# Down-projection of the MLP in three fp32r products with its split weights read back from DRAM, and nine MLP groups of two pieces

## What is computed

```python
scores = q @ k.T / sqrt(64)                      # 4 batches, 8 heads, 576 tokens, head size 64
kth = 32nd largest score of each row
scores = where(scores >= kth, scores, -1e9)
x = softmax(scores) @ v                          # laid out as 2304 tokens x 512
h = x @ w_in                                     # 512 -> 2048
g = max(h, 0) + log1p(exp(-abs(h)))              # softplus
x2 = g @ w_out                                   # 2048 -> 512
e = argmax(x2 @ w_gate); gate = softmax weight of e      # 8 experts
out = gate * (max(x2 @ w1[e], 0) @ w2[e])        # 512 -> 1024 -> 512
```

## Time and profile before

| | |
|---|---|
| Median of 3 runs | 1120.13 us (1118.76 to 1122.27) |
| Profiled execution, its own time / its span | 1119.99 us / 1118.3 us |
| Busy: PE, PEld (weight load), DVE, ACT, POOL | 1042.2, 761.5, 838.0, 658.8, 685.6 us |
| Mean granted clock of TensorE | 0.983 |
| HBM read / written | 40.12 MB / 9.70 MB |
| Mean of one: L737, L748, L754, L761 on ACT | 0.64, 0.78, 0.77, 0.69 us |
| Mean of one: L1308, L1312, L1320 (128x512) on POOL | 2.21, 1.42, 1.30 us |

### The profile page before, as it was taken

How to read it: one execution, slowest core, us unless ns; L and a number is a source line. 1 busy time by engine, 2 the same in 40 slices (tenths; PEclk the granted TensorE clock), 3 DMA queues, 4 the chain that set the end, 5 groups by cost and what they waited for, 6 DMA issues and landing times.

```text
span 1118.3 us, 20580 instructions
## 1 busy us (share of the span) xinstructions
PE 1042.2 (93%) x6728; PEld 761.5 (68%) x6729; DVE 838.0 (75%) x1838; ACT 658.8 (59%) x1313; POOL 685.6 (61%) x487
## 2 busy tenths in 40 slices
PE   3677679999999999999999999999999999999976
PEld 1455456777767767767767677677676788888864
DVE  7999998999999999999998999994036622222241
ACT  2677777777787787787777787786345111111130
POOL 4789997887887887887877788786121211112101
PEclk9879999999999999999999999999999999999989
DMA  9200011100011110000101000000314331111100
GB/s 336 92 1 1 1 52 44 43 21 1 1 29 56 43 42 1 1 20 1 58 29 62 2 1 20 1 1 20 151 40 158 127 120 48 38 38 47 38 9 19
DMA packets 26873, 50.71 MB, mean 45 GB/s; under 512 B 2656, under 2 KB 11872, under 8 KB 25760
## 3 DMA queue, kind: packets, MB, share of 16 engines
q1 hardware_dynamic: 23744, 39.87, 10.3%
q0 software_dynamic: 3040, 9.70, 2.4%
HBM read 40.12 MB, written 9.70 MB: 45 GB/s over the span
## 4 chain that ended last, share of the span: by engine, by line
PE 82%; DVE 11%; POOL 2%; ACT 2%; issue 1%; DMA 1%; DVEq 0%; POOLq 0%; SPq 0%; ACTq 0%
PE psum L531 20%; PE psum L478 8%; PE psum L443 7%; PE psum L603 7%; PE psum L513 6%; PE psum L604 6%; PE psum L605 6%; PE psum L460 6%; PE psum L515 5%; PE psum L517 5%; DVE top L976 5%; DVE work L982 4%; PE psum L552 2%; PE psum L632 1%; POOL pr L1308 1%
## 5 line engine op out<-in xcount | busy, mean ns | idle before, releaser
L1308 POOL TENSOR_SCALAR pr<-sc,top 128x576 f32<-128x576 f32 x144 | 318.7, 2213 | 38.3 <-DVE top L976 25.4
L976 DVE MAX8 top<-work 128x8 f32<-128x576 f32 x432 | 305.9, 752 | 0.0
L531 PE MATMUL psum<-wo,hT 128*128 128x512 f32 x576 | 272.3, 595 | 0.0
L982 DVE MATCH_REPLACE8 work<-top,work 128x576 f32<-128x576 f32 x288 | 212.5, 749 | 0.0
L1312 POOL TENSOR_TENSOR pr<-pr,sc 128x576 f32<-128x576 f32 x144 | 204.4, 1420 | 12.0
L1320 POOL TENSOR_TENSOR hT<-hs,ab 128x512 f32<-128x512 f32 (+1 forms) x80 | 95.0, 1187 | 151.4 <-ACT ab L807 151.3
L513 PE MATMUL psum<-x_hi,wi_hi 128*128 128x256 f32 x512 | 152.1, 297 | 0.8 <-ACT lg L833 0.7
L531 PEld LDWEIGHTS psum<-wo,hT 128*128 128x128 f32 x576 | 98.5, 191 | 68.4 <-issue 68.4
L515 PE MATMUL psum<-x_lo,wi_hi 128*128 128x256 f32 x512 | 144.6, 282 | 0.0
L517 PE MATMUL psum<-x_hi,wi_lo 128*128 128x256 f32 x512 | 144.5, 282 | 0.0
L460 PE MATMUL psum<-ident,pr 128*128 128x128 f32 (+1 forms) x720 | 105.4, 278 | 36.9 <-ACT prT L761 19.0
(11 more groups left out here) (184 smaller groups left out, 1659.7 us busy)
## 6 DMA issues: line engine op xcount, KB each, us to landing
wbuf<-in_moe_w SPq DMA_DIRECT2D x4, 2048.0 KB, 14.6
kT<-in_k SPq DMA_DIRECT2D x16, 288.0 KB, 3.0
qT<-in_q SPq DMA_DIRECT2D x16, 288.0 KB, 3.8
vtok<-in_v SPq DMA_DIRECT2D x16, 256.0 KB, 3.0
wi_raw<-in_moe_w_in SPq DMA_DIRECT2D x1, 4096.0 KB, 14.1
wo<-in_moe_w_out SPq DMA_DIRECT2D x1, 4096.0 KB, 24.6
x_rows<-x2tok SPq DMA_DIRECT2D x16, 256.0 KB, 2.2
wi_again<-in_moe_w_in SPq DMA_DIRECT2D x1, 4096.0 KB, 13.7
```

The costliest lines, as they stand in the source:

```text
L531: mm = nc.tensor.matmul(psum[:, 6 + a, :], hT[:, n % 4, part, a * P:(a + 1) * P], wo[:, f, :], start=(f == 0), stop=(f == KF - 1))
L976: nc.vector.max(top[:, at, 8 * r:8 * r + 8], sc[:, at, :] if r == 0 else work[:, t, :]).then_inc(topk_step, 1)
L982: nc.vector.match_replace(work[:, t, :], top[:, at, 8 * r - 8:8 * r], sc[:, at, :] if r == 1 else work[:, t, :], TAKEN).then_inc(topk_step, 1)
L1308: nc.gpsimd.tensor_scalar(pr[:, n % 2 * 2 + t, :], sc[:, at, :], top[:, at, TOPK - 1:TOPK], OUT, ALU.is_lt, ALU.mult).then_inc(mask_step, 1)
```

## The change

The down-projection becomes three fp32r products: the sum h is split into a high part (`h_high` on ScalarE) and a low rest (`h_low` on GpSimd), both in the step after, and w_out likewise. w_out is split in steps 1 to 4 (`split_wo`, `low_wo`), w_in now in steps 5 to 8, two units a step each. The split w_out goes to DRAM (`wo_parts`, 1 MB a unit) and comes back unit by unit into a ring of two (`load_wo`). The MLP has nine groups of two pieces, from step 10 on; eight of them run between the blocks, the ninth after them, and the steps end at 73 instead of 77. Of the masks, one tile of each even block, and both of the first eight blocks, get their comparison from a Relu on ScalarE (`cut_off`), and GpSimd only subtracts; the biases of the exponentials move from ScalarE to GpSimd. `reciprocals` come a block later on VectorE, behind the first maxima. In the last group the order of units, router and loads is new; the first expert's w1 and w2 go, in quarters, to where attention's buffers were, between the ring loads. Buffers move in SBUF, `up` uses one bank in the last group too, and the load `wi_again` falls away.

```diff
-    NA = NT - 1
+    NA = NT - 2
...
-    GROUPS = [[0]] + [[2 * g - 1, 2 * g] for g in range(1, NT // 2)] + [[NT - 1]]
+    GROUPS = [[2 * g, 2 * g + 1] for g in range(NT // 2)]
     LASTG = len(GROUPS) - 1
-    MLP_AT = 6
...
+    MLP_AT = 2 * PAIRS + 2
+    WIDE = 2 * P
...
+    FREE = MLP_AT - 2
+
+    def cuts(n):
+        return (0, 1) if n < FREE else ((0,) if n % 2 == 0 else ())
+
+    def tiles_of(n):
+        return (0, 1) if len(cuts(n)) != 1 else (1, 0)
+
+
+
+    def wo_units(i):
+        return range(2 * (i - 1), 2 * i) if 1 <= i <= UNITS // 2 else ()
+
+    def wi_units(i):
+        return wo_units(i - UNITS // 2)
...
+    wo_parts = nc.dram_tensor("wo_parts", (UNITS, P, 2, 2, DM), F32, kind="Internal").ap()
...
+            sp.dma_start(wo_raw[:], w_out.rearrange("(k p) n -> p k n", p=P)).then_inc(wo_loaded, 16)
             sp.dma_start(wi_raw[:], w_in.rearrange("(k p) f -> p k f", p=P)).then_inc(wi_loaded, 16)
-            sp.dma_start(wo[:], w_out.rearrange("(k p) n -> p k n", p=P)).then_inc(wo_loaded, 16)
             sp.dma_start(wg[:], w_gate.rearrange("(k p) e -> p k e", p=P)).then_inc(wg_loaded, 16)
 
+            def store_wo(u):
+                sp.wait_ge(wo_split, u + 1)
+                sp.dma_start(wo_parts[u], wo_ring[:, u % 2]).then_inc(wo_stored[u % 2], 16)
+
+            def load_wo(n):
+                if n < 2:
+                    for slot in range(2):
+                        sp.wait_ge(wo_stored[slot], 16 * UNITS // 2)
+                else:
+                    sp.wait_ge(h_used, n - 1)
+                sp.dma_start(wo_ring[:, n % 2], wo_parts[n % UNITS]).then_inc(wo_ready[n % 2], 16)
+
             for i in range(TAIL):
+                if up_at(i):
+                    load_wo(UNITS * up_at(i)[0] + up_at(i)[1])
...
+                for u in wo_units(i):
+                    store_wo(u)
...
+            first = UNITS * LASTG
+            for u in range(2):
+                load_wo(first + u)
...
+            for u in range(4, 8):
+                for n in ((0, 1) if u < 6 else ()):
+                    at = slice((u - 4) * 512, (u - 3) * 512)
+                    half = slice(n * KD // 2, (n + 1) * KD // 2)
+                    sp.dma_start(w1_to[:, half, at], w1_from[:, half, at]
+                                 ).then_inc(w1_first if u == 4 else w1_loaded[0], 16)
+                for n in ((0, 1) if u >= 6 else ()):
+                    at = slice((2 * (u - 6) + n) * KE // 4, (2 * (u - 6) + n + 1) * KE // 4)
+                    sp.dma_start(w2_to[:, at, :], w2_from[:, at, :]
+                                 ).then_inc(w2_first if u == 6 else w2_loaded[0], 16)
+                load_wo(first + u)
+            for a in range(2):
+                store_piece(2 * LASTG + a)
...
             def down(g, u, part):
                 n = UNITS * g + u
                 if part == 0:
                     pe.wait_ge(h_ready, n + 1)
-                    if n == 0:
-                        pe.wait_ge(wo_loaded, 16)
+                    pe.wait_ge(wo_ready[n % 2], 16 * (n // 2 + 1))
                     if u == 0 and g:
-                        pe.wait_ge(y_copied, turns_before(g))
+                        pe.wait_ge(y_copied, 2 * g)
                 f = 2 * u + part
-                for a in range(len(GROUPS[g])):
-                    mm = nc.tensor.matmul(psum[:, 6 + a, :], hT[:, n % 4, part, a * P:(a + 1) * P],
-                                          wo[:, f, :], start=(f == 0), stop=(f == KF - 1))
+                here = wo_ring[:, bass.ds(slots[n % 2], 1)].bitcast(F32R)
+                hi, lo = here[:, 0, 0, part, :], here[:, 0, 1, part, :]
+                for a in range(2):
+                    h_at = (n % 2, part, slice(a * P, (a + 1) * P))
+                    high, low = h_hi[:, h_at[0], h_at[1], h_at[2]], h_lo[:, h_at[0], h_at[1], h_at[2]]
+                    nc.tensor.matmul(psum[:, 6 + a, :], high, hi, start=(f == 0), stop=False)
+                    nc.tensor.matmul(psum[:, 6 + a, :], high, lo, start=False, stop=False)
+                    mm = nc.tensor.matmul(psum[:, 6 + a, :], low, hi, start=False, stop=(f == KF - 1))
                 if part == 1:
...
             up(LASTG, 1)
...
+            turn_tokens(LASTG - 1, NT - 4, 0)
+            turn_tokens(LASTG - 1, NT - 3, 1)
+            last_down(0)
+            logits(NT - 4, 2)
+            logits(NT - 3, 3)
             up(LASTG, 2)
+            last_down(1)
+            count_early()
             up(LASTG, 3)
-            count_early()
-            last_down(1)
...
+            last_down(2)
+            up(LASTG, 4)
+            last_down(3)
+            up(LASTG, 5)
             slots_early()
+            last_down(4)
+            up(LASTG, 6)
+            last_down(5)
             up(LASTG, 7)
-            last_down(5)
             last_down(6)
             pe.wait_ge(tables_ready, 1)
             rank_first = rank_at(0)
             turn_xs(0, 0)
             last_down(7)
...
+            e_up(0, rank_first, {(0, 2): lambda: turn_tokens(LASTG, NT - 2, 5),
+                                 (0, 3): lambda: turn_tokens(LASTG, NT - 1, 4),
+                                 (1, 1): lambda: logits(NT - 2, 3),
+                                 (1, 2): lambda: logits(NT - 1, 7)}, halves=True)
...
+            def cut_off(n, t):
+                act.wait_ge(limit_ready, sum(1 for x in range(n + 1) if cuts(x)))
+                if n >= 2:
+                    act.wait_ge(transit_full, 2 * (n - 2) + t + 1)
+                nc.scalar.activation(pr[:, n % 2 * 2 + t, :], sc[:, n % 3 * 2 + t, :], ACT.Relu,
+                                     bias=bias[:, n % 2, 1, t:t + 1], scale=-FAR).then_inc(cut, 1)
+
+            def exponentials(n, x):
+                t = tiles_of(n)[x]
                 act.wait_ge(bias_ready, n + 1)
-
...
-            def exponentials(n, t):
-                act.wait_ge(masked, 2 * n + t + 1)
+                act.wait_ge(masked, 2 * n + x + 1)
...
+            def h_high(g, u):
+                n = UNITS * g + u
+                act.wait_ge(h_summed, n + 1)
+                if n >= 2:
+                    act.wait_ge(h_used, n - 1)
+                nc.scalar.copy(h_hi[:, n % 2], hs[:, n % 2]).then_inc(h_high_ready, 1)
+
+            def split_wo(u):
+                act.wait_ge(wo_loaded, 16)
+                if u >= 2:
+                    act.wait_ge(wo_stored[u % 2], 16 * (u // 2))
+                nc.scalar.copy(wo_ring[:, u % 2, 0].bitcast(F32R), wo_raw[:, 2 * u:2 * u + 2, :]
+                               ).then_inc(wo_hi_ready, 1)
...
-                if late:
-                    normalise(i - 2, 0)
-                    normalise(i - 2, 1)
+                if up_at(i - 1):
+                    h_high(*up_at(i - 1))
                 if is_block(i + AHEAD):
                     scores_out(i + AHEAD, 0)
                     scores_out(i + AHEAD, 1)
                 if now:
-                    biases(i - 1)
-                    exponentials(i - 1, 0)
+                    for t in cuts(i - 1):
+                        cut_off(i - 1, t)
+                if late:
+                    normalise(i - 2, 0)
+                    normalise(i - 2, 1)
                 if up_at(i):
                     rectify(*up_at(i))
                 if late:
                     probs_out(i - 2, 0)
-                if up_at(i):
-                    logarithm(*up_at(i))
-                if up_at(i - 1) and up_at(i - 1)[0] == 0:
-                    split_wi(up_at(i - 1)[1])
+                if now:
+                    exponentials(i - 1, 0)
                 if late:
                     probs_out(i - 2, 1)
                 if i in TURNS:
                     turn_out(TURNS[i][1], 5)
+                if up_at(i):
+                    logarithm(*up_at(i))
                 if now:
                     exponentials(i - 1, 1)
+                for u in wo_units(i):
+                    split_wo(u)
+                for u in wi_units(i):
+                    split_wi(u)
                 if down_at(i) and down_at(i)[1] == UNITS - 1:
...
-                if is_block(n - 1):
-                    reciprocals(n - 1)
+                    if r == 0 and is_block(n - 2):
+                        reciprocals(n - 2)
...
+            def biases(n):
+                at = slice(n % 3 * 2, n % 3 * 2 + 2)
+                pool.wait_ge(topk_step, STEPS * (n + 1))
+                if n >= 2:
+                    pool.wait_ge(exp_ready, 2 * (n - 1))
+                if cuts(n):
+                    nc.gpsimd.tensor_scalar(bias[:, n % 2, 1, :], top[:, at, TOPK - 1], FAR, None,
+                                            ALU.mult).then_inc(limit_ready, 1)
+                nc.gpsimd.tensor_scalar(bias[:, n % 2, 0, :], top[:, at, 0], -1.0, None,
+                                        ALU.mult).then_inc(bias_ready, 1)
+
             def mask(n, t):
                 at = n % 3 * 2 + t
-                pool.wait_ge(topk_step, STEPS * n + STEPS - 2 + t + 1)
```

(49 more changed lines are left out.)

326 lines of the change are left out of this document (149 added, 177 removed).

## The result

The changed kernel takes 1138.0 us, median of 4 runs (1137.7 to 1139.4), against 1121.0 for the kernel before on the same chip (4 runs, 1118.8 to 1122.3): a ratio of 1.0157, interval 1.0137 to 1.0176. It is slower, as forecast (1137). The profiled execution took 1137.8 us with a span of 1136.0, where before the span was 1118.3.

What follows compares the result with a forecast made beforehand. TensorE bounds (82% of the last path), VectorE and GpSimd within 1.1 us. 1120.0 + (810.9 - 813.1) + (58.5 - 40.5) + 1.3 = 1137.1 us, forecast 1137; own range 1120 to 1150, overall 1098 to 1150.

Steps and rivals of the forecast that it cites:

- Part 1: Down-projection in fp32r on TensorE: 2.80 us a unit for 3.53, 0.73 less per step; steps 11 to 73 626 us.
- part 2: Main phase: new chain between ScalarE and GpSimd makes a pair of steps 21.1 us, steps 11 to 73 665 us.
- rival A: Main phase: VectorE sets the pace, steps 11 to 73 take 626 us, end at 1098; chance 0.21.
- Part 3: Start: weight splits lengthen the first steps, 12.9 us each for six; step 11 comes at 138, 20.6 us later.
- The sentence on the clock's worth: Start: with TensorE at 2.4 GHz throughout, it would be 2.7 us shorter and the end 1134.
- Rival B: Start also keeps VectorE's pace: 20 us less again, end at 1078; chance 0.04.
- Part 4: Ring loads of split weights: 5 us each, covered by more than 10 us, so they cost nothing.
- Rival C: Ring loads or stores come late, or the last units wait for weights behind the expert's quarters: 1150; chance 0.09.
- Part 5: End: from the last group's start to the first expert product 58.5 us, where it took 40.5.
- the wait for the gather: Last group: first gather on GpSimd behind h_low of the last unit but one, 0.7 us, at most 4.
- The first expert product's second piece: After the last group: a second piece in the first expert product adds 1.3 us.
- Rival D: Down-projection products miss the fp32r rate with a register in the address: 5.1 us a unit, some 1200; chance 0.01.

Runs made afterwards that it cites:

- experiment 4: Changed kernel without the low part of h (no GpSimd subtraction, third product takes the high part again): 1109.7 us, 0.9887 of the kernel before.
- Experiments 2: Changed kernel with one mask tile cut by ScalarE in every later block instead of every second: 1115.6 us, 0.9953 of the kernel before.
- 3: Changed kernel with no mask tile cut by ScalarE after the first eight blocks: 1156.9 us, 1.0323 of the kernel before.
- 8: Changed kernel with one down-projection product (high times high) in place of three: 1139.2 us, 1.0159 of the kernel before.
- experiment 7: Changed kernel with idle TensorE transposes ahead of the first up-projection, biases not moved: 1137.8 us, 1.0136 of the kernel before.
- experiment 6: Changed kernel with biases ahead of the splits' low parts and idle TensorE transposes at the start: 1122.7 us, 1.0014 of the kernel before.
- experiment 5: Changed kernel without 70 of the 72 ring loads of split w_out: 1118.8 us, 0.9974 of the kernel before.

## Why the prediction was right

**Part 1** held in its mechanism, not in its size: the fp32r products run at 0.233 us, but the first behind a set of transposes and the last ahead of one take 0.31, so that half a down-projection is 1.55 us and not 1.40. With the two sets of transposes it is 4.09 us (433.97 to 438.06) for 4.62 before, 0.53 less a step and not 0.73. It cost the main phase nothing, since the chain of part 2 bounds there. With that chain cut open (experiment 4) steps 11 to 73 fall to 635 us, at VectorE's pace. The bound was set 9 us too low at 626, so rival A as I priced it, 1098, would have come at about 1107.

**Part 2** held and carries the result. Forecast were 11.05 and 10.06 for the two kinds of step, measured 10.94 and 9.96, a pair 20.9 for 21.1; steps 11 to 73 took 660.7 for 665. Experiments 2, 3, 4 and 8 show it from four sides: a cheaper mask, a dearer mask, a link taken out, and a TensorE with less to do. Each of the first three moved the step as the chain says, the fourth moved nothing. The pair, 0.2 too long 31 times, makes 6.5 us too many; the steps with turned tokens and the batch ends took 12.8 us on top where I had 10.75, so that 4 remain. Rival A failed on the odd step, as was said against it.

**Part 3** gave the right sum for the first eight steps (biases at 123.45 for 123.0) with two errors against each other. The stores, for which I let step 2 wait until 45.6, cost 1.37 us there, and its biases came at 44.4. A split step is 13.17, not 12.9: from the normalisation until the first transposed tile is copied it is 2.18 us for my 1.7 (98.72 to 100.90 on ScalarE), from there to the first split 3.53 for 3.2, so the low clock costs 0.81 in the two transposes, not 0.45. Steps 9 and 10 took 19.9 us for my 15. Product with v, scores and the first up stand in line there (129.48, 132.01 and 134.15 on TensorE's timeline), product and scores at the low clock, which is 2.1 of the 4.9 us; the rest was not followed. So the mark of step 11 was 143.3 for 138, and the first scores of step 11 came at 143.0 where I had named 137. The sentence on the clock's worth, 2.7 us, is not borne out: alone it is worth nothing measurable (experiment 7), behind the first gate 8.3 (experiment 6). Rival B, a start at VectorE's pace, was out as said; but the order of splits, biases and cut, which spoke against it, is only 7 of the 20 us, the rest is the loop behind it at half clock and the wait for the stores.

**Part 4** held: TensorE's waits in the changed kernel hold none for a ring load, and experiment 5 brings no mark forward. Rival C is out.

**Part 5**: the last group started at 811.9 for 810.9 and took 59.96 for 58.5. The term that was too small is the wait for the gather, 3.15 + 0.32 where I had 0.7, and behind it the last down-projection, 4.43 us from 867.43 to 871.86 where 2.80 was counted, part of it at a low clock behind that wait (granted 0.62 from 869 to 872). That is 4.4 us more in the two; the other terms of the group came out 2.9 us shorter than I had them. The first expert product's second piece, for which I added 1.3, cost nothing: the tail is 0.6 shorter.

**Rival D** is out by the down rows above. The sum, 1137.1 for 1137.8, is better than its parts, and that is luck: +5 at the start, -4 in the main phase, +1.5 and -1.9 at the end. That the change makes the kernel slower, and by the chain of part 2, is not luck.

## What to carry to other kernels

Moving work from the engine that bounds to engines with time to spare is worth what the chain between those engines allows, and that chain is counted per iteration, from one instruction round to itself: 10.45 us a plain step on the mean here, against 9.61 of TensorE's own (experiment 4). When a step alternates between a cheap and a dear form, the dear one sets the loss, and one line that makes all steps the cheap form took all of it back. Read an experiment that changes data by marks inside the trace: one run was 19 us shorter, by other routing of the tokens, and had no step shorter.
